# Two moves between partitions in a three-stage kernel: ReLU rows without DRAM, gathered rows turned in 32x32 squares

## What is computed

```python
for e in range(E):
    mask = expert_idx == e
    h = np.maximum(x[mask] @ w1[e], 0.0)
    out[mask] = gate_w[mask, None] * (h @ w2[e])
```

## Time and profile before

| what | value |
|---|---|
| median of 3 runs | 805.91 us |
| lowest and highest run | 804.76 and 806.39 us |
| the profiled execution, its own time | 806.47 us |
| its span | 804.7 us |
| TensorE busy in the span | 98% |
| VectorE, ScalarE, GpSimd busy | 57%, 42%, 26% |
| instructions | 17127 |

### The profile page before, as it was taken

The page is one execution under the profiler, slowest core; times in us unless marked ns, Lnnn a source line. Parts: engine busy times, 40 slices in busy tenths (PEclk is TensorE's granted clock), DMA queues, the critical chain, the costliest instruction groups (busy, mean ns, idle before and its releaser), DMA issues.

```text
span 804.7 us, 17127 instructions
## 1 busy us (share of the span) xinstructions
PE 790.6 (98%) x5025; PEld 685.8 (85%) x5026; DVE 457.6 (57%) x721; ACT 341.8 (42%) x625; POOL 211.2 (26%) x281
## 2 busy tenths in 40 slices
PE   8999999999999999999999999999999999999998
PEld 7888887988989889989888888888888888888987
DVE  7899987786567476565565444433524434434332
ACT  3554554565446356444354334333423432433323
POOL 6666632233343243232124003001200400100100
PEclk9999999999999999999999999999999999999999
DMA  9987764766886877977652203203202102100301
GB/s 233 278 253 235 224 224 164 251 213 241 295 281 206 321 229 277 307 212 275 233 72 40 40 18 102 39 1 98 60 0 78 40 0 58 60 1 21 98 1 40
DMA packets 77394, 117.04 MB, mean 145 GB/s; under 512 B 34855, under 2 KB 58963, under 8 KB 77344
## 3 DMA queue, kind: packets, MB, share of 16 engines
q1 hardware_dynamic: 68096, 101.33, 41.0%
q0 software_dynamic: 5952, 15.04, 5.7%
q10 hardware_dynamic: 3296, 0.06, 0.2%
HBM read 83.02 MB, written 34.78 MB: 146 GB/s over the span
## 4 chain that ended last, share of the span: by engine, by line
PE 63%; DMA 18%; SPq 7%; issue 7%; DVE 2%; POOL 1%; ACT 0%; DVEq 0%; ACTq 0%; POOLq 0%
PE bank L1819 24%; PE bank L1880 20%; DMA hidden_rows<-hs 15%; PE bank L1870 4%; SPq L445 3%; PE bank L1600 3%; PE bank L1638 3%; PE bank L1617 2%; DMA qkas<-qka 2%; PE bank L1772 2%; PE bank L1792 2%; SPq L482 2%; PE bank L1646 1%; DMA hds<-hidden_rows 1%; SPq L620 1%
## 5 line engine op out<-in xcount | busy, mean ns | idle before, releaser
L1819 PE MATMUL bank<-yT,wts 128*128 128x512 f32 x864 | 204.5, 390 | 0.3 <-DVE g L1374 0.3
L1819 PEld LDWEIGHTS bank<-yT,wts 128*128 128x128 f32 x864 | 162.0, 188 | 34.0 <-DVE g L1374 0.7
L1880 PE MATMUL bank<-gs,wts 128*128 128x512 f32 x720 | 169.7, 389 | 0.0
L1880 PEld LDWEIGHTS bank<-gs,wts 128*128 128x128 f32 x720 | 135.1, 188 | 28.1
L1374 DVE TENSOR_TENSOR g<-bank,small 128x512 f32<-128x512 f32 x96 | 65.9, 687 | 149.1 <-ACT small L981 146.5
L1772 PE MATMUL bank<-wts,gxT 128*128 (+1 forms) x549 | 133.6, 396 | 0.2
L981 ACT ACTIVATE small<-bank 128x512 f32<-128x512 f32 x96 | 57.2, 596 | 166.9 <-PE bank L1819 159.9
L1772 PEld LDWEIGHTS bank<-wts,gxT 128*128 128x128 f32 x549 | 100.8, 188 | 21.7 <-issue 1.6
L1566 DVE TENSOR_TENSOR gs<-g,gs 128x512 fp32r<-128x512 f32 x96 | 66.5, 692 | 66.8 <-ACT gs L1087 66.1
L1087 ACT ACTIVATE gs<-g 128x512 fp32r<-128x512 f32 x96 | 60.8, 633 | 82.7 <-DVE g L1374 72.8
L829 POOL DMA_INDIRECT out<-os,tokens x20 | 19.7, 985 | 287.3 <-ACT os L1076 282.7
(11 more groups left out here) (190 smaller groups left out, 836.6 us busy)
## 6 DMA issues: line engine op xcount, KB each, us to landing
raw<-weights SPq DMA_DIRECT2D x60, 512.0 KB
hidden_rows<-hs SPq DMA_DIRECT2D x29, 512.0 KB
hds<-hidden_rows SPq DMA_DIRECT2D x29, 512.0 KB
qkas<-qka SPq DMA_DIRECT2D x20, 675.5 KB, 5.2
vs<-v SPq DMA_DIRECT2D x24, 192.0 KB, 4.0
x_rows<-xs SPq DMA_DIRECT2D x24, 192.0 KB, 4.0
yl<-y_rows SPq DMA_DIRECT2D x20, 192.0 KB, 5.0
x_rows<-raw SPq DMA_DIRECT2D x20, 192.0 KB, 3.2
```

The lines of the kernel that those rows point to most:

```text
L1819: m = pe.matmul(gps[f % 2][:, :], wts[:, 0, w_part, n:n + P], yT[:, 1 - u, y_part, k], start=(k == 0 and (w_part, y_part) == (0, 0)), stop ...
L1880: m = pe.matmul(out_turned[u][k][:, :], wts[:, 1, w_part, n:n + P], gs[:, f % 4, g_part], start=(f == 0 and (w_part, g_part) == (0, 0)), s ...
```

## The change

Three things are changed. First, the ReLU rows `hs` are moved to `hds` by four transfers within SBUF, one for each 32 partitions of `hs`, and the scratch rows in DRAM are dropped; the one wait ahead of them is for the remainder of block m-2. Second, for blocks from 5 on VectorE transposes the 32x32 squares of the gathered rows, `xg` to `xq`, right after its `gx_rest` of the block before, SyncE moves `xq` to `xd` by four transfers at the start of `move`, and ScalarE and VectorE split `xd` into `gxT`; `turn_gx` is left out. Third, the features are assigned to partitions in another order: partition p holds rows 3p, 3p+1 and 3p+2 of w1 (the array is laid out so on the host), and the transposes that stay on TensorE read every third column of `xg`. `xd` lies in the memory of `yf`, `xq` in that of `os`. GpSimd's gathers wait for the new semaphore where the block is turned by VectorE.

```diff
@@ build
+        x_squared = sem("x_squared")
+        x_moved = [sem(f"x_moved{j}") for j in range(2)]
+        SQUARED = 5
+        def x_passed(w, u):
+            return (w * 8 - 8 * (SQUARED - 2) - 8 * (1 - u)) * QUADS
+        def x_square(ap):
+            return ap.rearrange("p (k i t) -> p k i t", i=QUADS, t=SQ)
+        def x_in_place(u):
+            return xd[:, u].rearrange("p (i k t) -> p k i t", i=QUADS, t=SQ)
+        def squared(w):
+            return not isinstance(w, int) or w >= SQUARED
         def passed(w, u):
-            return w * 8 - 8 * u
+            return (w * 8 - 8 * u) * QUADS
@@ block.sync
+            def move_x(w, u):
+                if not squared(w) or isinstance(w, int) and w >= WINDOWS:
+                    return
+                sp.wait_ge(x_squared, w - SQUARED + 1)
+                for i in range(QUADS):
+                    sp.dma_start(xd[:, u, i * PIECE:(i + 1) * PIECE], xq[i * SQ:(i + 1) * SQ, u]).then_inc(x_moved[u], 16)
             def move(w, u):
                 due = sets_due(w)
+                move_x(w + 2, u)
                 load_next(due, 0)
                 sp.wait_ge(h_turned, w * 2 - 2 * FIRST + 2)
                 if not (isinstance(w, int) and w < FIRST + 2):
-                    sp.wait_ge(h_moved[u], passed(w, u) - 16)
-                sp.dma_start(h_rows[u], hs[:, u]).then_inc(h_stored[u], 16)
+                    sp.wait_ge(ht_lo, w * 2 - 2)
+                for i in range(QUADS):
+                    sp.dma_start(hds[:, u, i * QF:(i + 1) * QF], hs[i * SQ:(i + 1) * SQ, u]).then_inc(h_moved[u], 16)
                 load_next(due, 1)
-                sp.wait_ge(h_stored[u], passed(w, u))
-                if not (isinstance(w, int) and w < FIRST + 2):
-                    sp.wait_ge(ht_lo, w * 2 - 2)
-                sp.dma_start(hds[:, u].rearrange("p (i n) -> p i n", i=QUADS), h_quarters[u]).then_inc(h_moved[u], 16)
                 load_next(due, 2)
@@ block.gpsimd
+            def rows_read(w):
+                if squared(w):
+                    pool.wait_ge(x_squared, w - SQUARED + 1)
+                else:
+                    pool.wait_ge(gx_turned, w + 1)
...
-                        pool.wait_ge(gx_turned, first_gather + n - 1)
+                        rows_read(first_gather + n - 2)
@@ block.scalar
             def gx_round(w, u):
-                act.wait_ge(gx_turned, w + 1)
-                act.activation(gxT[:, u, 0], gxps, ACT.Copy).then_inc(gx_hi, 1)
+                if not squared(w):
+                    act.wait_ge(gx_turned, w + 1)
+                    act.activation(gxT[:, u, 0], gxps, ACT.Copy).then_inc(gx_hi, 1)
+                    return
+                act.wait_ge(x_moved[u], x_passed(w, u))
+                act.wait_ge(h_ready, w * 2 - 2)
+                act.activation(x_square(gxT[:, u, 0]), x_in_place(u), ACT.Copy).then_inc(gx_hi, 1)
@@ block.vector
+            def turn_x(w, u):
+                dve.wait_ge(gathered[u], w // 2 * 16 + 16 if isinstance(w, int) else w * 8 + (16 - 8 * u))
+                if not (isinstance(w, int) and w < SQUARED + 2):
+                    dve.wait_ge(x_moved[u], x_passed(w, u) - 16 * QUADS)
+                dve.transpose(xq[:, u].rearrange("p (n f) -> p n f", f=SQ),
+                              xg[:, u].rearrange("p (f n) -> p n f", f=SQ)).then_inc(x_squared, 1)
             def gx_rest(w, u):
                 dve.wait_ge(gx_hi, w + 1)
-                dve.tensor_tensor(gxT[:, u, 1], gxps, gxT[:, u, 0].bitcast(F32), ALU.subtract).then_inc(gx_lo, 1)
+                if squared(w):
+                    dve.tensor_tensor(x_square(gxT[:, u, 1]), x_in_place(u), x_square(gxT[:, u, 0].bitcast(F32)),
+                                      ALU.subtract).then_inc(gx_lo, 1)
+                else:
+                    dve.tensor_tensor(gxT[:, u, 1], gxps, gxT[:, u, 0].bitcast(F32), ALU.subtract).then_inc(gx_lo, 1)
+                if ahead(w, 1) and squared(w + 1):
+                    turn_x(w + 1, 1 - u)
@@ block.vector, turn_h
-                        dve.wait_ge(h_stored[u], passed(w, u) - 16)
+                        dve.wait_ge(h_moved[u], passed(w, u) - 16 * QUADS)
@@ block.tensor
             def turn_gx(w, u):
...
-                    m = pe.transpose(gxps[:, k * P:(k + 1) * P], xg[:, u, k * P:(k + 1) * P], ident[:, :])
+                    m = pe.transpose(gxps[:, k * P:(k + 1) * P], xg[:, u, k::KD], ident[:, :])
...
-                    if rows_first(w) and ahead(block, 1):
+                    if rows_first(w) and ahead(block, 1) and not squared(block + 1):
                         turn_gx(block + 1, 1 - at)
@@ kernel
-    w1 = moe_w1[:, features].reshape(E, D // 128, 128, F).transpose(0, 2, 1, 3).reshape(E, 1, 128, -1)
+    w1 = moe_w1[:, features].reshape(E, 1, 128, -1)
```

More of the change, by code:

```diff
@@ L23, with build @@
 AX = mybir.AxisListType
-def build(nc, qka, v, emb, tau, weights, x_dram, y_dram, gate_dram, h_dram, out):
+def build(nc, qka, v, emb, tau, weights, x_dram, y_dram, gate_dram, out):
     P = 128
@@ L73, in build @@
     QF = F // QUADS
-    h_rows = [h_dram[u * P:(u + 1) * P] for u in range(2)]
-    h_quarters = [r.rearrange("(i f) (j n) -> (f j) i n", i=QUADS, j=QUADS) for r in h_rows]
     gate_rows = gate_dram.rearrange("(b c p) k -> b p c k", c=CH, p=P)
@@ L214, in build @@
             yl = sb("yl", [P, 2, GT // SQ, PIECE])
+            yf_at = (nc.sbuf_base + 31) // 32 * 32
             yf = sb("yf", [P, 2, GT])
+            assert 2 * D <= 2 * GT
             seat(TO_W_IN)
@@ L221, in build @@
             hds = nc.alloc_sbuf_tensor_at("hds", [P, 2, F], F32, offset=yT_at)
+            xd = nc.alloc_sbuf_tensor_at("xd", [P, 2, D], F32, offset=yf_at)
             hr = nc.alloc_sbuf_tensor_at("hr", [P, 2, HALF], F32, offset=yT_at + 2 * F * 4)
@@ L228, in build @@
             hT_odd = nc.alloc_sbuf_tensor_at("hT_odd", [P, 2, F], F32R, offset=os_at)
-            assert 2 * F <= 2 * TG * D
+            xq = nc.alloc_sbuf_tensor_at("xq", [P, 2, D], F32, offset=os_at + 2 * F * 4)
+            assert 2 * F + 2 * D <= 2 * TG * D
             tokens = sb("tokens", [P, TILES - TG, YW - D])
@@ L321, in build @@
         h_turned = sem("h_turned")
-        h_stored = [sem(f"h_stored{j}") for j in range(2)]
         h_moved = [sem(f"h_moved{j}") for j in range(2)]
@@ L1740, in turn_first @@
                 for k in range(KD):
-                    pe.transpose(gx_first[k], xg[:, 0, k * P:(k + 1) * P],
+                    pe.transpose(gx_first[k], xg[:, 0, k::KD],
                                  ident[:, :]).then_inc(first_turned if k < KD - 1 else gx_turned, 1)
@@ L1975 @@
     scratch = [nc.dram_tensor(n, (rows, w), F32).ap()
-               for n, rows, w in (("x_rows", B * S, H * HD), ("y_rows", 2 * B * S - 512, H * HD + 4), ("token_gates", B * S, 4),
-                                ("hidden_rows", 256, F))]
+               for n, rows, w in (("x_rows", B * S, H * HD), ("y_rows", 2 * B * S - 512, H * HD + 4), ("token_gates", B * S, 4))]
     out = nc.dram_tensor("out", (B * S, moe2_w_out.shape[1]), F32, kind="ExternalOutput").ap()
```

## The result

The changed kernel is slower: median 842.76 us (840.06 to 845.04, four runs), beside 805.34 (803.74 to 806.39, four runs) for the kernel before. The ratio is 1.0479, 95% interval 1.0456 to 1.0502. Forecast were 795.6 us, at most 802.4. The profiled execution took 842.23 us, its span is 840.4.

The account below looks back on a forecast made before the run. TensorE, busy 98% of the span, was taken as the bound, with SyncE's late queue second. 7.5 (turns removed) + 1.1 + 2.1 + 0.7 - 1.0 - 0.1 = 10.3 us below 805.91 gave 795.6 us, range 791.5 to 802.4.

Parts of the forecast that it names:

- ReLU rows in one hop: SyncE's queue: four 128 KB transfers replace store and load; the hop is covered, gaining 2.1 us and 0.7 us.
- What is added: New work: VectorE transpose 0.57 us a block within its idle time, SyncE's x transfers 1.3 us, remaining turns 0.1 us.
- the loop of x: VectorE transpose, SyncE issues, hop, split, next transpose: at least 3.2 us plus landing time, which may average 5.1 us.
- bursts are absorbed mostly: x behind weights in SyncE's queue: about 6.5 us of slack, 1.0 us of new stalls, bounds 0 and 6.
- The gain: Whole kernel: 10.3 us saved, from 805.91 to 795.6 us.
- the 2.8 us that SyncE's lateness was to give back: TensorE's even stretch: 2.1 us from late start and a shorter wait, 0.7 us from small sequencer waits.
- the early windows: Turns 5 to 7 gain nothing as VectorE is late; the next hidden product starts at 183.8 against 184.94: 1.1 us.
- the late start at the end: TensorE's contraction at 394.34 instead of 392.62, from SyncE running late: 1.7 us that would go.
- (c): Rival: x stands behind weights and ReLU rows, landing averages 6.2 us, windows take 9.4 us: 816 us, chance 0.07.
- (d): Rival: the four x quarters move one after another, 8.0 us, windows take 9.9 us: 828 us, chance 0.03.

Follow-up runs that it names:

- e13: Changed kernel, its eight quarter transfers a window kept, but each landing on the same 32 partitions in long rows (products of other numbers): 846.17 us, ratio 1.0526.
- e11: Changed kernel with x and ReLU rows each moved by one straight transfer over all 128 partitions (squares change no partition): 806.21 us, ratio 1.0040.
- e16: Changed kernel with only the ReLU rows moved in one straight transfer, x left in quarters (ReLU squares change no partition): 819.77 us, ratio 1.0206.
- e15: Changed kernel with GpSimd issuing the four x transfers, VectorE turning x before the remainder, and the gather a block earlier: 812.9 us, ratio 1.0115.
- e4: Changed kernel with SyncE sending the next block's x ahead of the second and third weight pieces: 827.11 us, ratio 1.0290.
- e3: Changed kernel with each weight piece loaded in the windows cut to an eighth of its columns, number of loads kept: 823.21 us, ratio 1.0249.
- e12: e11 with x ahead of two weight pieces, VectorE's turn before the remainder, and the gather a block earlier: 799.84 us, ratio 0.9949.
- e1: Changed kernel with the x part undone (TensorE turns every gathered block), ReLU rows still in one hop: 803.35 us, ratio 1.0001.
- e6: Changed kernel with VectorE turning x of the next block before the remainder of the current one: 840.27 us, ratio 1.0440.
- e10: Changed kernel with the orders of e4 and e6 and the gather a block earlier, all quarters still by SyncE: 827.47 us, ratio 1.0292.
- e17: e15 with the squares only from block 9 on, TensorE turning blocks 0 to 8: 800.01 us, ratio 0.9955.
- e5: Changed kernel with ScalarE instead of SyncE issuing the four x transfers, between its two ReLU halves: 839.3 us, ratio 1.0419.

## Why the prediction was wrong

**The step that failed** is SyncE's in "ReLU rows in one hop" and "What is added": "loses the 3.8 us wait and one issue of 0.37, gains three of 0.33", and four x transfers at "4 x 0.33 = 1.3 us". The price came from a store to DRAM of 512 KB. A quarter within SBUF costs 0.60, so the window has 4.8 us of such issues, not 8 x 0.33 = 2.6. By the prediction's prices SyncE would be 1.9 us a window freer than before (0.7 + 3.8 against 2.6); it is 0.3 us fuller. A nearer row was at hand: the prediction took the landing of the quarters of out_rows, also read from 32 partitions, but not their issue. Kernel before (ns min/median/max, first and last start):

```profile
L667 SPq DMA_DIRECT2D x_rows<-raw x20: 315/516/897, 480.3 to 742.9; - x20
```

At 0.52 the eight would have made 4.1 us, and the relief 0.4. And the term was put only into the loop of x; SyncE's own time in a window (weights, table reads, eight issues) was never summed against 8.29. Even at 0.33 that sum should have stood there. e13 shows that the number of issues alone makes the loss, e11 and e16 that it goes with the number; e15 that it goes, but for the start, when half of them leave SyncE (and x, by that, leaves its place behind the weights too, so e15 takes away both parts at once).

**The second step** is "bursts are absorbed mostly", with 1.0 us of new stalls (bounds 0 and 6). TensorE stalled for 31.9. The slack of 6.5 us was counted for x alone. In the window above SyncE's lateness of 6.5 us takes all of it before the first quarter is issued, and then come the bytes of the weights (15 to 18 us by e4 and e3). And a third thing was not in the sum at all: ScalarE waits for x in front of ReLU, so that a late x of one block delays a bank that another block needs.

**The gain** was too large as well. Even e12, which has neither the issues nor the order in the way, is only 4.0 us faster than the kernel before (803.84 to 799.84), not 10.3. Two terms account for that roughly: the 2.8 us that SyncE's lateness was to give back, which e1 does not show, and the early windows. There the hidden product that started at 175.47 in the kernel before starts at 178.21 in e12 and at 177.61 in the kernel after, behind a wait of 3 us for VectorE's `gxT`, and the next at 187.28 in e12, not at 183.8: 3.5 us. VectorE was late there, as the prediction saw. That the added transpose made it later was not tested by itself.

**The clock** had no term. 13.1 us are products that ran slowly after a stall.

**What was right.** L1748 has 12 matmuls left (L1797), the window is 8.28, the wait for the store is gone, ScalarE's `gxT` waits for `xd`, and the late start at the end is gone: the last contractions of the even stretch follow one another without a gap in the kernel after. The transpose took 870 ns, not 570, within the bound of 1.1. The span of e1's profile is 4.4 us shorter than that of before, but the kernel before itself spread from 801.05 to 805.65 on that chip, and the two medians agree.

**The rivals.** (c), the hop loop binds, foresaw the sign and the first symptom, with a chance of 0.07 and 816 us. Its condition isn't what happened: it wanted a landing later than 5.8 us after the last issue in the mean, and in the kernel after it was 2.6, once above 5.8. But its loop did run longer than a window: 0.87 + 2.5 + 2.6 + 0.52 + 0.56 + 0.3 and 2.5 us of waiting for SyncE, for which the prediction's loop had no term, make 9.9, and the transposes of blocks 6 to 30 followed each other at 9.96. Opening that loop (e6, and e10 over e4) brought 3 us at most, since SyncE's own step was about as long (9.0 us by the estimate above). (d), quarters in turn, is not supported: in the window read from e3 the last of four quarters had landed 1.5 us after its issue, where (d) counted 6.7. As for the sentence of the Trainium skill (SBUF — State Buffer, "Can I just issue two DMAs to hit both halves?"), that one transfer over 128 partitions beats several, it holds in effect (e11 against the kernel after, 806 and 843 us), though e13 shows the price in the issuing queue. Whether the data of the quarters move in turn, no run here shows.

**Open.** Why a quarter within SBUF takes 0.60 us to issue, when a store to DRAM takes 0.33 and a transfer over all partitions 0.47: e13 excludes short rows and the change of partitions, and the 0.52 of L667 shows that DRAM as the target isn't what makes an issue short, no more. How the loss splits between ReLU rows and x beyond e16: x alone in one transfer was not run. And whether e17's order with SyncE in GpSimd's place would do: not run.

## What to carry to other kernels

A queue that issues transfers is an engine: before one transfer is cut into four, sum all its issues of a window, each at the duration of its own kind, and hold that against the window; where no row of that kind exists, take the nearest in shape (here one that also reads 32 partitions), and the dearest as the bound. A wait that disappears from a queue is no gain if issues of the same length take its place. Look who stands behind each new wait in program order (here ReLU behind the split of x), since a stall of a few microseconds can cost TensorE its clock as well (13.1 of 45.0 us here); and let a deeper pipeline begin after the crowded start.

## What the runs showed of the hardware

- Median issue time differed by the kind of transfer: 0.33 us (512 KB, SBUF to DRAM), 0.37 (back), 0.52 (from 32 partitions to DRAM, 192 KB, L667 before), 0.47 to 0.51 (within SBUF, 128 partitions, 192 or 512 KB, e11 and e16), 0.60 (within SBUF, from 32 partitions, 48 or 128 KB). 48 and 128 KB cost the same, and SyncE (0.60), ScalarE (0.63, e5) and GpSimd (0.60, e15) nearly so.
- After eight of ten stalls of 2.4 to 8.6 us (kernel after, e15, and one in e12) the next product of TensorE took 5.8 to 7.3 us in place of 4.3; around four of them in the kernel after the mean granted clock of 20 us was 0.83. The other two, both of 3 us, left it at 4.4.
- VectorE's transpose of 128x384 with its source read at a stride of 48 bytes took 870 ns, that of 128x512 at stride one 688 in the same kernel: 1.7 times as much per element.
- Loading weights for TensorE with every third float of a row took 199 ns in e1 where the contiguous 128x128 took 139 before; the matmuls stayed at 278 against 272.
